# The first FFN takes all four H banks in turn also in the first four slots of step 1

## The reference

```python
s = kn.transpose(0, 2, 1) @ qn / tau      # qn, kn: q, k normalised over the tokens
x = v @ softmax(s)                        # 6016 x 256

h = x @ w_in                              # first FFN, 256 -> 2048
P = a[0] + a[1]*h + a[2]*h**2 + a[3]*h**3
Q = 1 + |b[0]|*|h| + |b[1]|*h**2
y = (P / (Q + 1e-6)) @ w_out              # 2048 -> 256

h = y @ w_in2                             # second FFN
out = (h * clip(h + 3, 0, 6) / 6) @ w_out2
```

## Time and profile before

| | us |
|---|---|
| median of 3 runs | 1125.63 (1124.23 to 1125.67) |
| the profiled execution | 1124.4 |
| its span, first to last instruction | 1122.6 |
| TensorE busy in it | 1097.7 (98%) |
| VectorE busy | 901.0 (80%) |
| ScalarE busy | 868.9 (77%) |
| GpSimd busy | 781.2 (70%) |
| mean granted TensorE clock | 0.995 of full |

### The profile page before, as it was taken

One profiled execution on the slowest core, in us unless ns is written; L12 is line 12 of the kernel. 1 busy time (PEld: TensorE's weight loads), 2 busy tenths in 40 slices (PEclk: granted clock), 3 DMA queues, 4 the chain that ended last, 5 costly groups with the idle time before them and its releaser, 6 DMA issues.

```text
span 1122.6 us, 16081 instructions
## 1 busy us (share of the span) xinstructions
PE 1097.7 (98%) x5004; PEld 921.3 (82%) x5004; DVE 901.0 (80%) x1286; ACT 868.9 (77%) x1468; POOL 781.2 (70%) x625
## 2 busy tenths in 40 slices
PE   9978799999999999999999999999999999999998
PEld 8877688888888888888888888888888888888887
DVE  6689999987887887887897888788798788787632
ACT  6698888877877877787887777877777787777643
POOL 0278889777776777776777776777777677776643
PEclk9999899999999999999999999999999999999999
DMA  9931010010010020020020020010011010010010
GB/s 351 294 128 20 0 20 1 15 19 1 10 30 1 0 39 1 0 38 0 0 38 0 1 38 0 0 32 6 1 22 17 1 20 1 1 20 1 1 19 20
DMA packets 105465, 33.82 MB, mean 30 GB/s; under 512 B 92982, under 2 KB 98742, under 8 KB 105398
## 3 DMA queue, kind: packets, MB, share of 16 engines
q1 hardware_dynamic: 104832, 32.52, 11.6%
q10 hardware_dynamic: 566, 0.52, 0.1%
HBM read 26.87 MB, written 6.16 MB: 29 GB/s over the span
## 4 chain that ended last, share of the span: by engine, by line
PE 91%; DVE 5%; ACT 1%; issue 1%; DMA 0%; POOL 0%; SPq 0%; DVEq 0%; ACTq 0%
PE H L447 15%; PE H L448 14%; PE H L449 14%; PE YP L449 7%; PE YP L448 7%; PE YP L447 7%; PE OP L449 7%; PE OP L448 7%; PE OP L447 7%; PE OP L480 3%; DVE SQ L926 1%; DVE H L911 1%; DVE g_hi L919 1%; DVE T L904 1%; PE OP L618 1%
## 5 line engine op out<-in xcount | busy, mean ns | idle before, releaser
L401 POOL TENSOR_TENSOR SQ<-SQ,AB 128x512 f32<-128x512 f32 (+1 forms) x192 | 247.6, 1290 | 256.4 <-ACT SQ L721 256.0
L415 POOL TENSOR_TENSOR g_lo<-R,g_hi 128x512 fp32r<-128x512 f32 (+1 forms) x191 | 243.4, 1274 | 28.8 <-ACT g_hi L753 28.8
L407 POOL TENSOR_TENSOR g_lo<-SQ,Y 128x512 fp32r<-128x512 f32 (+1 forms) x192 | 244.7, 1274 | 6.2 <-DVE SQ L934 6.2
L719 ACT ACTIVATE AB<-H,absb 128x512 f32<-128x512 f32 (+1 forms) x192 | 130.4, 679 | 144.9 <-PE H L449 144.9
L904 DVE TENSOR_TENSOR T<-T,H 128x512 f32<-128x512 f32 (+1 forms) x192 | 128.9, 672 | 85.4 <-ACT T L727 85.4
L919 DVE SCALAR_TENSOR_TENSOR g_hi<-H,coef,Y 128x512 fp32r<-128x512 f32 (+1 forms) x192 | 141.6, 737 | 53.7 <-ACT Y L740 51.3
L447 PE MATMUL H<-vT_hi,wf_hi 128*128 128x512 f32 (+1 forms) x384 | 150.3, 392 | 14.6 <-DVE wf_lo L891 8.8
L926 DVE SCALAR_TENSOR_TENSOR SQ<-SQ,g_hi 128x512 f32<-128x512 f32 (+1 forms) x192 | 155.7, 811 | 6.6
L940 DVE SCALAR_TENSOR_TENSOR R<-R,H 128x512 f32<-128x512 f32 (+1 forms) x192 | 128.1, 667 | 35.2 <-ACT R L746 35.2
L746 ACT ACTIVATE R<-H 128x512 f32<-128x512 f32 (+1 forms) x192 | 113.4, 591 | 51.7 <-PE H L449 50.9
L447 PE MATMUL YP<-g_hi,wd_hi 128*128 128x512 f32 (+1 forms) x384 | 149.6, 390 | 3.5 <-POOL g_lo L407 3.3
(11 more groups left out here) (104 smaller groups left out, 2054.0 us busy)
## 6 DMA issues: line engine op xcount, KB each, us to landing
qk<-in_q SPq DMA_DIRECT2D x22, 256.0 KB, 5.2
qk<-in_k SPq DMA_DIRECT2D x22, 256.0 KB, 6.1
v_blocks<-in_v SPq DMA_DIRECT2D x88, 64.0 KB, 2.3
out<-o_tok SPq DMA_DIRECT2D x80, 64.0 KB, 1.9
wd_raw<-in_moe_w_out SPq DMA_DIRECT2D x8, 512.0 KB, 9.2
w_raw_a<-in_moe_w_in SPq DMA_DIRECT2D x2, 1024.0 KB, 10.7
wu_raw<-in_moe_w_in SPq DMA_DIRECT2D x4, 512.0 KB, 6.2
qk<-in_q SPq DMA_DIRECT2D x3, 128.0 KB, 3.0
```

Source lines behind the costliest of these rows:

```text
L401: nc.gpsimd.tensor_tensor(SQ[:, j % 4, 0:w], SQ[:, j % 4, 0:w], AB[:, j % 2, 0:w], ALU.add)\
L407: nc.gpsimd.tensor_tensor(g1_lo[:, j % 4, 0:w], SQ[:, j % 4, 0:w], Y[:, j % 2, 0:w], ALU.mult)\
L415: nc.gpsimd.tensor_tensor(g2_lo[:, j % 4, 0:w], R[:, j % 2, 0:w], g2_hi[:, j % 4, 0:w].bitcast(fp32), ALU.subtract).then_inc(g2_lo_done, 1)
```

## The change

In slots 16 to 19 the first FFN's chunks take bank j mod 4 instead of j mod 2, that is banks 0, 1, 2, 3 for (1,0) to (1,3); from (1,4) on banks 0 and 1 in turn as before. The waits follow the new holders: up1(1,0) to up1(1,3) wait for rest of (0,12) to (0,15) (before: (0,12), (0,13), (1,0), (1,1)), up1(1,4) and up1(1,5) for rest of (1,0) and (1,1) (before: (1,2), (1,3)), and up2(0,0) and up2(0,1) for rest of (1,2) and (1,3) (before: (0,14), (0,15)). All other waits, the instructions and their order on each engine stay.

```diff
+    assert SHIFT2 == 4
...
         def h1(t, j):
-            turn = 4 if isinstance(t, int) and t == 0 else 2
-            return H[:, j % turn, 0:width(t)]
+            all_four = slot(t, j) is not None and slot(t, j) < J + 4
+            return H[:, j % (4 if all_four else 2), 0:width(t)]
 
         def wait_h1(engine, t, j):
             if isinstance(t, int) and t == 0:
                 if j >= 4:
                     wait_chunk(engine, rest_done, (0, j - 4))
-            elif isinstance(t, int) and t == 1 and j < 2:
-                wait_chunk(engine, rest_done, (0, J - 4 + j))
+            elif isinstance(t, int) and t == 1 and j < 6:
+                wait_chunk(engine, rest_done, back(t, j, 4))
             else:
                 wait_chunk(engine, rest_done, back(t, j, 2))
...
         def wait_h2(engine, blk, j):
             if isinstance(blk, int) and blk == 0 and j < 2:
-                wait_chunk(engine, rest_done, (0, J - 2 + j))
+                wait_chunk(engine, rest_done, (1, 2 + j))
```

## The result

The changed kernel takes 1126.78 us in the median of 22 runs (1125.29 to 1127.53), the kernel before 1124.68 in 22 runs beside it (1124.17 to 1125.67). The ratio is 1.0015, 95% interval 1.0009 to 1.0022: slower by 1.0 to 2.5 us. The medians are less than 0.2% apart, the bound from which the prediction calls a kernel slower. Of the first three runs of before, two had been high, so the forecast of 1127.6 stood on a base 0.95 us too high; its difference, +2.0, is close to the measured one (+2.1 by the medians). The profiled execution of the changed kernel took 1127.06 us around a span of 1125.2. Its file has one line more ahead of L443, so every line of the page after is one higher than before (L948 of before is L949).

The account below looks back on a forecast made before the run. TensorE alone bounds from the entry (140.81 us) on, VectorE paces the stretch before. (a) 0, (b) +1.1, +0.9 and +0.1, (c) 0, taken as +2.0: 1127.6 us, range 1124.3 to 1129.6.

Parts of the forecast that it names:

- The entry decides: Start of step-1, chunk-6 up projection (140.81 us before): TensorE alone bounds from there; the kernel's end moves exactly as much.
- the 142.5 to 143.2 that was named: Sign to look for in the trace: the time in us at which the entry would come.
- (a): up1(1,2), up1(1,3) in banks 2 and 3: hole moves before down1(1,0), products spend VectorE's 1.3 us lead; 0 (-1.4 to +0.4).
- (b): up2(0,0), up2(0,1) wait for rest(1,2), rest(1,3), delaying c1(0,0): +1.1 wait, +0.9 low clock, +0.1 groups behind up2(0,1).
- the wait that was named there: Sign at up2(0,1): TensorE waits there for SQ of L934, that is for rest(1,3).
- (c): up1(1,4), up1(1,5) wait for the long-done rest(1,0), rest(1,1) but stand behind up2(0,0), up2(0,1): gain nothing, 0.
- Nothing moves: Rival: the later up2 is absorbed because VectorE paced 127 to 141 us anyhow; 0, 1125.6 us; chance 0.10.
- faster: Rival: VectorE's 1.31 us reach the entry, both products free and clock full; -1.4, 1124.2 us; chance 0.07.
- One more product: Rival: product(1,3) is caught by GpSimd too, 1.1 more at up2(0,1) and entry; +3.1, 1128.7 us; chance 0.13.
- Half the price, by the clock: Rival at up2(0,0): clock already full there (or product(1,2) ahead of wd_lo); only +1.1, 1126.7 us; chance 0.25.
- The rule that was weighed: Skill's thin matmul kernel: PSUM double-buffering gave no further gain once loops were right; alone it gives 0, 1125.6 us.

Follow-up runs that it names:

- e4: Kernel before plus 22 small matmuls of ones in TensorE's gap ahead of up1(1,2); +2.7 us against before.
- e7: Changed kernel with c1 (ScalarE) and gate2 (VectorE) of slots 20 and 21 behind all first-FFN work there; +6.2 us against before.
- e5: e2 plus 26 small matmuls of ones in TensorE's gap and one weight-split piece in slot 20 instead of 19; 1123.25 us, ratio 0.9989 against before.
- e11: e9 with, in slots 20 and 21, c1 behind root and root_squared and gate2 behind rest; +0.1 us against before.
- e8: Changed kernel with one piece of the second FFN's down weight split in slot 20 instead of 19; +1.1 us against before.
- e1: Kernel before with only the new waits: up2(0,0) and up2(0,1) wait for rest(1,2) and rest(1,3), banks stay two; +1.5 us against before.
- e9: Changed kernel plus small matmuls of ones in both TensorE gaps, 26 before down1(1,0) and eight before up2(0,0); +1.8 us against before.
- e2: Changed kernel with chunks (1,2) and (1,3) in OP's two idle banks and the old waits at up2(0,0) and up2(0,1); +0.4 us against before.
- e3: Changed kernel plus 26 small matmuls of ones in TensorE's gap before down1(1,0); +1.5 us against before.
- e13: e9 with one piece of the second FFN's down weight split in slot 20 instead of 19; +1.1 us against before.

## Why the prediction was right

*The entry decides.* Right: the span less the entry is 981.67 to 981.79 in ten of the fourteen profiles, and where it is more TensorE is held up behind the entry: by 3.3 us in e4, 2.4 in e7, and 0.3 in e5 and e11, start to start. All of the loss is at the entry: 143.52 - 140.81 = 2.71 us, of which 0.40 had come up ahead of product(1,0), leaving 2.31 where +2.1 was worked out. Seen in the trace the entry is at 143.52, outside the 142.5 to 143.2 that was named; with the 0.40 taken off it is at 143.12.

*(a), the hole is moved and the lead is spent.* Right, step by step. AB(1,2) came at 121.46 and q_body(1,2) at 123.11, both with the 0.4 of shift taken off within 0.1 of the forecast. Product(1,1) took 1.11 and product(1,2) 1.60 us. Rest(1,2) started at 130.35, that is 0.15 us early by the yardstick, where 0.05 was said. e8 shows that the second of these collisions is worth 0.9 at the entry.

*(b), c1 behind the new wait.* Right in its place and near in its size. ScalarE's wait was 5.29 us (4 to 5 said) and c1(0,0) 2.08 later by the yardstick (+2.0 said). By e1 and e9 it splits as worked out: about 1.2 for the wait at full clock (1.1 said) and 0.93 for the clock (0.9 said). Up2(0,1) came 3.33 later (3.2 said).

What the prediction had wrong in detail is the length of the low clock. It lasted to 136.4, for 8.7 us of TensorE's time after the gap and not 6.2, so that up1(1,4) and down1(1,1) were slow as well. AB(1,4) waited 0.89 for TensorE, and TensorE reached up2(0,1) at 137.50 just as rest(1,3) ended (136.70 + 0.75), so the wait that was named there does not show. In the second profile of the change the clock was back 15.27 us behind product(1,0) instead of 16.71; there the wait shows with 0.55, and up2(0,1) and the entry are at the same place within 0.02 us. So the extra length cost nothing. TensorE is its own bound from up2(0,1) on: to the entry it took 6.02 us (5.9 said).

That the clock was low at up2(0,0) is right for both profiles of the change, and in part luck. The prediction took it from the 6.2 us of before; in e7 the same gap left the clock full 0.36 us ahead of up2(0,0).

*(c)* Nothing, as said.

*The rivals.* "Nothing moves" and "faster" are out by the interval. "One more product" did not come: product(1,3) and (1,4) took 0.69. "Half the price, by the clock" is not fully out: e7's profile shows that the clock can be full at up2(0,0), and the six runs of the change at a mean clock of 0.997 are only 1.0 us above before. How many executions are of this kind is not known.

*The rule that was weighed* (the Trainium skill, TensorE: Matmul & The Clock Gate, section "HAM oscillation — how this bites in real kernels") would have given 0. That more banks bring no gain held even with the wait left out (e2, +0.4, whose interval holds zero). The change as it stands costs 2.1 us, and there the measurement decides.

## What to carry to other kernels

A buffer that is lent from one stage to another brings its wait along: look at what stands behind the first instruction of the lender in every in-order queue, not only on the engine that gets the buffer. Before a gap is closed, find the engine that paces the stretch and ask how much of the gap is its own idle time (here 1.31 of 5.10 us for VectorE), and whether a faster neighbour will collide with it. Where one engine is full without a gap to the end, the start of that stretch is a yardstick that measures to a tenth of a microsecond what medians cannot.

## What had not been expected of the hardware

In e3 the granted clock fell to half at 131.2, right behind a gap of TensorE of 1.84 us that followed small matmuls and down1(1,0). In the kernel before a gap of 1.65 us, ended at 111.30, passed without a fall. With eight small matmuls in the place of e3's gap, the clock stayed full from 115 to 145 us (e9).

Two stops of TensorE of 1.6 and 1.2 us without a semaphore came up in the loop, in the middle of the span, in the one profile with 44 instructions more ahead of it (e4), and none in the profiles with 52 (e3, e5) or 68 more (e9, e11, e13). An edit of TensorE's list can cost more in another place than it brings in its own: e4 had its entry 1.24 us earlier and was 2.7 us slower.

A product of two SBUF operands on VectorE, 512 columns wide, took 0.69 us in all 2019 cases of the fourteen profiles in which no GpSimd operation was running at its start. In 384 of the 445 others it ended 0.55 us after the GpSimd operation did, and took 0.71 to 1.80 us. In the last 61 the operation had less than 0.1 us left: the product took 0.69 in 60 of them and 1.84 in one. The Trainium skill states this contention (GPSIMD Engine Reference, section "Key points": VectorE instructions with two SBUF inputs contend with GpSimd); by the products of these traces it agrees.
